# Running the first tile of expert 0 on batch 0's tokens while batch 1 is routed, and leaving the dummy matmuls out of the routing

## The reference

```python
# 1. windowed attention: 2 batches, 8 heads, 768 tokens, head size 64; keys 0..7 and the last 96 are kept
a = softmax(scale * q @ k.T - slope * dist, keep);  x = (a @ v) as [2, 768, 512]
# 2. mixture of 8 experts, one expert a token
for b in range(2):
    for s in range(768):
        fresh_e = argmax(x[b, s] @ w_gate)
        e = fresh_e if s == 0 or sigmoid(x[b, s] @ w_local) < 0.5 else prev_e
        prev_e = e
        out[b, s] = softmax(x[b, s] @ w_gate)[e] * (relu(x[b, s] @ w1[e]) @ w2[e])   # 512 -> 1024 -> 512
# 3. real part of a 2-D FFT of x added to x, layer norm, 512 -> 2048 -> 512 with relu, residual
```

## Time and profile before

| | |
|---|---|
| median of 3 timed runs | 678.57 us (677.31 to 679.86) |
| the profiled execution, its own time | 677.65 us |
| its span | 675.8 us |
| PE busy | 649.7 us, 96% of the span |
| VectorE, ScalarE, POOL busy | 317.0, 207.5, 213.7 us |
| share of PE in the chain that ended last | 85% |
| mean granted TensorE clock | 0.987 of full speed |

### The profile page before, as it was taken

One profiled execution on the slowest core, in us unless ns is written; L12 is line 12 of the kernel. 1 busy time (PEld: TensorE's weight loads), 2 busy tenths in 40 slices (PEclk: granted clock), 3 DMA queues, 4 the chain that ended last, 5 costly groups with the idle time before them and its releaser, 6 DMA issues.

```text
span 675.8 us, 10507 instructions
## 1 busy us (share of the span) xinstructions
PE 649.7 (96%) x3372; PEld 530.2 (78%) x3373; DVE 317.0 (47%) x828; ACT 207.5 (31%) x410; POOL 213.7 (32%) x120
## 2 busy tenths in 40 slices
PE   8999999769999999999998989999999999999997
PEld 7777878658888888888875668888888888888886
DVE  4999787574635446345347845441221111311112
ACT  3666544303332432433204752132211122111110
POOL 0000001235778777999515646270000000000000
PEclk9999999879999999999999989999999999999999
DMA  8664347226657556678255033210010000100001
GB/s 300 245 223 165 130 132 283 81 114 236 212 166 270 191 188 243 219 243 272 64 182 163 17 125 124 94 32 0 1 62 1 1 0 1 63 0 1 0 1 62
DMA packets 35409, 82.91 MB, mean 123 GB/s; under 512 B 3362, under 2 KB 7714, under 8 KB 35364
## 3 DMA queue, kind: packets, MB, share of 16 engines
q1 hardware_dynamic: 17952, 40.46, 16.8%
q10 hardware_dynamic: 15492, 35.56, 15.9%
q0 software_dynamic: 1920, 6.29, 2.8%
HBM read 67.35 MB, written 14.94 MB: 122 GB/s over the span
## 4 chain that ended last, share of the span: by engine, by line
PE 85%; DVE 9%; issue 2%; DMA 2%; ACT 1%; POOL 0%; DVEq 0%; ACTq 0%; POOLq 0%; SPq 0%
PE psum L597 22%; PE psum L599 22%; PE psum L598 22%; PE psum L1888 5%; PE psum L1860 3%; PE psum L1871 2%; PE psum L2036 2%; PE psum L1798 2%; PE psum L1996 1%; DVE prob L1407 1%; DMA bounds_i<-in_n_local 1%; PE psum L1792 1%; DVE prob_t L1421 1%; PE psum L2117 1%; DMA u<-y_sorted,result_rows 1%
## 5 line engine op out<-in xcount | busy, mean ns | idle before, releaser
L722 POOL TENSOR_TENSOR w<-raw,w 128x1024 fp32r<-128x1024 f32 x56 | 132.5, 2398 | 40.0 <-ACT w L820 39.8
L1752 DVE SCALAR_TENSOR_TENSOR act_t<-psum,act_t 128x512 fp32r<-128x512 f32 x48 | 33.2, 691 | 191.6 <-ACT act_t L1102 191.6
L820 ACT ACTIVATE w<-raw 128x1024 fp32r<-128x1024 f32 x64 | 67.3, 1058 | 123.9 <-PE psum L599 55.7
L1102 ACT ACTIVATE act_t<-psum 128x512 fp32r<-128x512 f32 x48 | 28.7, 598 | 217.8 <-PE psum L599 217.8
L597 PE MATMUL psum<-un_t,wc 128*128 128x512 f32 x192 | 75.5, 393 | 1.4 <-DVE un_t L1676 1.4
L597 PE MATMUL psum<-wc,act_t 128*128 128x512 f32 x192 | 75.6, 394 | 0.0
L599 PE MATMUL psum<-un_t,wc 128*128 128x512 f32 x192 | 75.4, 393 | 0.0
L598 PE MATMUL psum<-un_t,wc 128*128 128x512 f32 x192 | 75.2, 392 | 0.0
L599 PE MATMUL psum<-wc,act_t 128*128 128x512 f32 x192 | 74.8, 390 | 0.0
L598 PE MATMUL psum<-wc,act_t 128*128 128x512 f32 x192 | 74.8, 389 | 0.0
L874 ACT ACTIVATE prob<-prob,top 128x256 f32<-128x256 f32 (+1 forms) x96 | 46.2, 482 | 48.1 <-DVE top L1407 47.7
(11 more groups left out here) (273 smaller groups left out, 1109.9 us busy)
## 6 DMA issues: line engine op xcount, KB each, us to landing
raw<-in_moe_w ACTq DMA_DIRECT2D x60, 512.0 KB, 4.3
k_win<-in_k SPq DMA_DIRECT2D x8, 768.0 KB, 5.6
raw<-in_moe_w_ch SPq DMA_DIRECT2D x12, 512.0 KB, 3.3
v_win<-in_v SPq DMA_DIRECT2D x8, 704.0 KB, 4.2
xs<-x_sorted SPq DMA_DIRECT2D x17, 256.0 KB, 4.6
y_sorted<-ys SPq DMA_DIRECT2D x16, 256.0 KB, 3.4
q_t<-in_q SPq DMA_DIRECT2D x8, 384.0 KB, 3.5
out<-u SPq DMA_DIRECT2D x12, 256.0 KB, 2.0
```

The costliest lines, as they stand in the source:

```text
L722: nc.gpsimd.tensor_tensor(w[:, slot, 1, m, at_:at_ + PIECE], raw[:, n % RING, :], w[:, slot, 0, m, at_:at_ + PIECE].bitcast(f32), ALU.subt ...
L820: nc.scalar.activation(w[:, slot, 0, m, at_:at_ + PIECE], raw[:, n % RING, :], ACT.Copy).then_inc(high_done, 1)
L1102: nc.scalar.activation(act_t[n % 2][:, 0, :], bank(act_bank(n)), ACT.Relu).then_inc(act_high, 1)
L1752: nc.vector.scalar_tensor_tensor(act_t[n % 2][:, 1, :], bank(act_bank(n)), 0.0, act_t[n % 2][:, 0, :].bitcast(f32), ALU.max, ALU.subtract) ...
```

## The change

The first tile of the expert part is no longer "the first 128 tokens of expert 0", known once both batches are routed, but "the first tokens of batch 0 for expert 0, up to 128". They are known when batch 0 is routed, still during attention. `x_sorted` gets a block of 128 rows ahead of all areas for them; batch 0's scatter puts them there, and SP loads them as soon as batch 0's scatter is done. The remaining tokens of expert 0 begin a tile of their own. All the work of that tile then stands between the stages of batch 1's routing, and its first steps are done by ACT (`first_tile_high`, `first_tile_hidden`) and VectorE (`first_tile_low`, `first_tile_rest`) at fixed places. The 25 dummy matmuls around the routing are left out.

```diff
 # place(b), for b == 0
+link(tensor_scalar(in_first_tile, slot_f[:, these], 2.0 * P, float(P), ALU.is_lt, ALU.mult))
+link(tensor_tensor(slot_f[:, these], slot_f[:, these], in_first_tile, ALU.subtract))
 tensor_copy(slots[:, these], slot_f[:, these]).then_inc(slots_ready, 1)
 link(tensor_tensor(area, row["area"], upto[0][:, :, ST - 1], ALU.add))
+link(tensor_tensor(area, area, row["first_row"], ALU.max))
+link(tensor_tensor(sorted_first, area, row["first_row"], ALU.subtract))
 # control
-link(v.tensor_tensor_scan(last_tile, ones[:, 0:E], tiles, 0.0, ALU.mult, ALU.add))
+link(v.tensor_tensor_scan(last_tile, ones[:, 0:E], tiles, 1.0, ALU.mult, ALU.add))
 ...
 link(v.tensor_tensor(base_row[:, :], base_row[:, :], count[:, :], ALU.add))
+first_tile_rest()
 # ACT
+def first_tile_high():
+    act.wait_ge(xs_turned, 1)
+    activation(xs_t[0] high, bank(4), ACT.Copy).then_inc(xs_t_high, 1)
+def first_tile_hidden():
+    for part in range(2):
+        act.wait_ge(hid_sum, part + 3)
+        activation(hid[0][:, part * 512:(part + 1) * 512], bank(part), ACT.Relu).then_inc(hid_ready, 1)
+    act.wait_ge(hid_turned, 1)
+    for z in range(2):
+        activation(hid_t high, quarter z, bank(2 + z), ACT.Copy).then_inc(hid_t_high, 1)
 # DVE
+def first_tile_low():      dve.wait_ge(xs_t_high, 1);      xs_t[0] rest <- bank(4) - high
+def first_tile_rest():     for z in range(2): dve.wait_ge(hid_t_high, z + 1);  hid_t rest <- bank(2 + z) - high
+def first_tile_result():   dve.wait_ge(mm2_parts, 2 * PARTS);  ys[0] <- bank(5)
-x_tile(0, 0)
+x_tile(1, 1)
+first_tile_result()
 share(1)
 first_results()
-x_tile(1, 1)
-rectify(0, 0, 0)
-rectify(0, 0, 1)
-tile_step(0, 0, 2)
-mirrored_rows()
+x_tile(2, 0)
+rectify(1, 1, 0)
+rectify(1, 1, 1)
 tile_step(0, 1, 2)
+mirrored_rows()
 # SP
-sp.wait_ge(rows_ready, 1)
-first_rows = [row_of(j) for j in range(2)]
 sp.wait_ge(heads_cleared, 16)
 sp.wait_ge(results_cleared, 16)
-sp.wait_ge(scattered, 16 * NT)
-for par in range(2):
-    load_tile(first_rows[par], par)
+sp.wait_ge(first_scattered, 16 * ST)
+sp.dma_start(xs[0][:, :], x_sorted[0:P, :]).then_inc(xs_loaded[0], 16)
+sp.wait_ge(rows_ready, 1)
+first_rows = [row_of(j) for j in range(1, 3)]
+sp.wait_ge(scattered, 16 * ST)
+load_tile(first_rows[0], 1)
 sp.wait_ge(xs_turned, 1)
-load_tile(row_of(2), 0)
+load_tile(first_rows[1], 0)
 # PE, end of attention and routing of batch 1
-for t in range(4):
+for t in (2, 3, 0, 1):
     sum_last(t)
 values(UNITS - 1)
 turn_x(len(X_FILLS) - 1)
+turn_tile(0, 0, 16)
 for t in range(4, ST):
     sum_last(t)
-for stage in (turn_flags, ends_to_row, carry_to_column, codes_to_columns, rank_tokens): stage(1)
-pe.wait_ge(slots_ready, 2);  keep_busy(7)
-pe.wait_ge(rows_ready, 1);   keep_busy(8)
-pe.wait_ge(ctl_ready, 1);    half, odd = loads of ctl
-keep_busy(7)
-turn_tile(0, 0, 16)
-keep_busy(3)
-first_up(0, 0)
+pe.wait_ge(xs_t_ready, 1)
+up(0, 0, 0, 0, range(NC - 1));  turn_flags(1);  up(0, 0, 0, 0, range(NC - 1, NC))
+ends_to_row(1);  up(0, 0, 1, 0, range(1))
+carry_to_column(1);  codes_to_columns(1);  rank_tokens(1)
+up(0, 0, 1, 0, range(1, NC))
+for z in range(2): pe.wait_ge(hid_ready, z + 1); 4 transposes of hid[0]
+for c in range(NF - 2): second_product(0, 0, c)
+pe.wait_ge(ctl_ready, 1)
 turn_tile(1, 1, 16)
-up(0, 0, 1, slot_of(0))
+for c in range(NF - 2, NF): second_product(0, 0, c)
+first_up(1, 1);  half, odd = loads of ctl
+turn_tile(2, 0, 32)
+up(1, 1, 1, slot_of(1))
 mirror_rows()
-first_up(1, 1)
-tile_step(0, 0, 2)
+first_up(2, 0)
 tile_step(0, 1, 2)
```

More of the change, by code:

```diff
@@ L911, in _ @@
             act.wait_ge(ctl_ready, 1)
-            for n in range(2):
-                act.wait_ge(xs_loaded[n], 16)
+            act.wait_ge(xs_loaded[1], 16)
+            act.wait_ge(xs_loaded[0], 32)
             expert(1, 1)
@@ L1845, in rank_tokens, with keep_busy, turn_tile @@
                 nc.tensor.matmul(BANK_TOTALS, ones[:, :], flags, start=True, stop=True).then_inc(ranks_ready, 1)
+            def keep_busy(n):
+                for _ in range(n):
+                    nc.tensor.matmul(bank(7)[:, 0:2 * P], ident, square[:, 0:2 * P], start=True, stop=True)
+            def turn_tile(j, par, count):
+                pe.wait_ge(xs_loaded[par], count)
+                if not (isinstance(j, int) and j == 0):
+                    pe.wait_ge(xs_t_ready, j)
+                for c in range(NC):
+                    ins = nc.tensor.transpose(bank(4)[:, c * P:(c + 1) * P], xs[par][:, c * P:(c + 1) * P], ident)
+                ins.then_inc(xs_turned, 1)
@@ new lines, in ready_of, with slot_of, weights, up @@
+            def ready_of(j):
+                return nc.tensor.value_load(ctl[0:1, ds(j, 1)], min_val=0, max_val=(E - 1) * WPIECES)
+            def slot_of(j):
+                return nc.tensor.value_load(ctl[0:1, ds(SLOTS + j, 1)], min_val=0, max_val=1)
+            def weights(slot, x, m, c0):
+                return w[:, ds(slot, 1), x, m, c0:c0 + 512].rearrange("p s n -> p (s n)")
+            def up(j, par, part, slot, chunks=range(NC)):
+                if not (isinstance(j, int) and j == 0):
+                    pe.wait_ge(hid_ready, 2 * j + part - 1)
+                for c in chunks:
+                    c0 = c * F + part * 512
+                    ins = three_passes(bank(part), xs_t[par][:, 0, c, :], xs_t[par][:, 1, c, :],
+                                       weights(slot, 0, 0, c0), weights(slot, 1, 0, c0), c == 0, c == NC - 1)
+                if NC - 1 in chunks:
+                    ins.then_inc(hid_sum, 1)
@@ new lines, in tile_step @@
+            def tile_step(p, par, ahead):
+                j = 2 * p + par
+                early = isinstance(j, int)
+                if ahead == 0:
+                    keep_busy(1)
+                pe.wait_ge(hid_ready, 2 * j + 2)
+                if not (early and j == 0):
+                    pe.wait_ge(hid_t_ready, 2 * j)
+                for c in range(NF):
+                    ins = nc.tensor.transpose(bank(2 + c // 4)[:, (c % 4) * P:(c % 4 + 1) * P],
+                                              hid[par][:, c * P:(c + 1) * P], ident)
+                ins.then_inc(hid_turned, 1)
+                if ahead == 0:
+                    keep_busy(3)
+                if ahead >= 1:
+                    slot = slot_of(j + 1)
+                if ahead >= 2:
+                    up(j + 1, 1 - par, 1, slot)
+                    turn_tile(j + 2, par, 16 * p + 32)
+                if ahead == 1:
+                    up(j + 1, 1 - par, 1, slot, range(NC // 2))
+                own_slot = slot_of(j)
+                pe.wait_ge(rest_done, ready_of(j) + WPIECES)
+                if not (early and j < 2):
+                    pe.wait_ge(ys_ready, j - 1)
+                for c in range(NF):
+                    if c % 4 == 0:
+                        pe.wait_ge(hid_t_ready, 2 * j + c // 4 + 1)
+                    second_product(par, own_slot, c)
+                if ahead >= 2:
+                    first_up(j + 2, par)
+                if ahead == 1:
+                    up(j + 1, 1 - par, 1, slot, range(NC // 2, NC))
@@ new lines, in _ @@
+                turn_tile(0, 0, 16)
+            pe.wait_ge(rest_done, WPIECES // 2)
+            pe.wait_ge(xs_t_ready, 1)
+            up(0, 0, 0, 0, range(NC - 1))
+            turn_flags(1)
+            up(0, 0, 0, 0, range(NC - 1, NC))
+            ends_to_row(1)
+            up(0, 0, 1, 0, range(1))
+            carry_to_column(1)
+            codes_to_columns(1)
+            rank_tokens(1)
+            pe.wait_ge(rest_done, WPIECES)
+            up(0, 0, 1, 0, range(1, NC))
+            for z in range(2):
+                pe.wait_ge(hid_ready, z + 1)
+                for c in range(4):
+                    ins = nc.tensor.transpose(bank(2 + z)[:, c * P:(c + 1) * P],
+                                              hid[0][:, (4 * z + c) * P:(4 * z + c + 1) * P], ident)
@@ L2065, in mirror_rows @@
+            ins.then_inc(hid_turned, 1)
+            for c in range(NF - 2):
+                if c % 4 == 0:
+                    pe.wait_ge(hid_t_ready, c // 4 + 1)
+                second_product(0, 0, c)
+            pe.wait_ge(ctl_ready, 1)
             def mirror_rows():
```

180 lines of the change are left out of this document (84 added, 96 removed).

## The result

| | before | changed |
|---|---|---|
| median of 20 runs each | 677.65 us (676.12 to 679.86) | 683.96 us (675.75 to 686.26) |
| profiled execution, its span | 677.65, 675.8 us | 683.4, 681.6 us |
| mean granted TensorE clock | 0.987 | 0.980 |
| PE busy; share in the chain | 649.7 us; 85% | 644.3 us; 80% |

The ratio is 1.0069, with an interval of 1.0050 to 1.0088: 0.7% slower, where 669.0 and faster was forecast, and above the range, which ended at 674. The ratio compares the means of the fast runs, so the three slowest of the changed kernel's 20, which count as slow, are not in it. PE is busy 5.4 us less, but the dummies in the routing alone had been 13.1 us of its busy time.

What follows compares the result with a forecast made beforehand. PE was taken to bound the kernel, with holes set by batch 1's routing chain on VectorE. The terms put the second tile's transposes at 169.25 against 178.56, 9.3 us earlier, giving 669.0 us, range 665.5 to 674.

Steps and rivals of the forecast that it cites:

- Attention: Four small VectorE steps added by place(0) during attention: cost 0 if hidden, 0.85 us if not, taken as 0.3.
- First tile there in time: End of attention: the first tile's load arrives at 128.5, 0.7 us before PE turns it at 129.2; lateness taken as 0.
- Ready at 131.3 ... Nothing lost: After attention: the first tile's input is ready at 131.3, just when the gate sums come, at no cost.
- Flags +1.1, ranks +0.8: Batch 1's routing: flags wait 0.3 to 2.1 us behind nine matmuls, taken as 1.1; ranks reach VectorE 0.8 later.
- Control held 2.65: VectorE behind base_row: waits for the first tile's hidden values, done at ranks (R) + 5.6, holding control 2.65 us.
- Behind control 5.75: From control's end at 153.2 to the second tile's first product: 5.75 us of VectorE's steps, loads and input copies.
- Rival (b): VectorE's work behind control doesn't hold PE; first product 3.9 us earlier, saved 13.2, 665.1 us; chance 0.05.
- First product to transposes 9.2 + 0.8: Second tile, first product to hidden-value transposes: 9.2 us of PE's work, plus 0.8 for the clock.
- Dummies 0 to 3.3, taken as 0.8: Second tile's first products: low clock without dummies costs 0, 1.6 or 3.3 us; taken as 0.8.
- Rival (a): The low clock stays through the routing and again at 159: saved 4.9 us, 673.6; chance 0.14.
- rival (c): Experts' weights lead: POOL's row sets the pace from expert 1 on and starts 1.0 later; 679.6 us; chance 0.03.
- rival (d): Splitting expert 0 makes a 17th tile if batch 0 has under 68 tokens for it: 681.6 us; chance 0.03.

Runs made afterwards that it cites:

- e4: The kernel before, with its 25 dummy matmuls in the routing left out: ratio 0.9999 to the kernel before.
- e5: The kernel before, with VectorE's share(1) and first_results moved behind x_tile(1, 1): ratio 1.0195 to the kernel before.
- e2: The changed kernel, with PE's nine first products and VectorE's first four routing stages put ahead of the jump: ratio 1.0061 to the kernel before.
- e3: The changed kernel with 21 dummy matmuls put back: ratio 1.0000 to the kernel before.
- e8: e1 with the work ahead of the jump as in e2 and the 21 dummies of e3: ratio 0.9892 to the kernel before.
- e6: The changed kernel, both shares moved into VectorE's wait for ACT, place_results and first_results behind the second tile's input: ratio 0.9900 to the kernel before.
- e1: The changed kernel, with POOL's weight subtractions made to wait for the last step of first_results: ratio 0.9913 to the kernel before.
- e7: e6 with the work ahead of the jump as in e2 and the 21 dummies of e3: ratio 0.9881 to the kernel before.

## Why the prediction was wrong, point by point

The sum was 9.3 us sooner at the transposes; it was 5.1 later. The 14.4 us between are these:

- **Attention**: 0.7 (128.78 to 129.48), where 0.3 stood: 0.4 more, within its ends of 0 to 0.85. Executions of the other kernels differ by more than this (t0 from 128.86 to 134.34), so no part of it can be put down to the change.
- **First tile there in time**: right. SP's load was issued at 126.15, and the transposes follow the last turn without a wait.
- **"Ready at 131.3 ... Nothing lost", "nine matmuls start at 131.5"**: the input was ready at 131.7, but PE began at 134.16. The term that is missing is the jump. It was in the kernel before too, and could not be seen there: VectorE's 2.58 us ahead of the gate sums are put down to PE, and I took them for PE's. But PE's last sum had ended at 130.71 and VectorE began at 131.31, 0.6 later. In e4 and e5 it ended 1.0 ahead of VectorE's start, and VectorE's stop was 2.58 again (rows of e4 below): it was not PE that it waited for last. By e2, all of VectorE's 2.18 us go with the place of the instructions, and of PE's stop 2.3 us, with 1.07 left at the flags. The Trainium skill (Runtime: NRT & Kernel Launch, "Instruction fetch mechanics") says that a taken branch out of the window of fetched code makes the engine wait for it; e2 agrees with that as to place, but no run here shows the fetch itself.
- **Flags +1.1, ranks +0.8**: ranks came at 142.18, where 139.4 (with attention's 0.3) stood: 2.8 late, of which attention 0.4, the jump about 2, the rest the half clock on the nine products. They took 3.2 us (134.16 to 137.33), and 1.1 of wait was the middle between full and half. By e3, the clock alone is 1.0 there. So the 0.4 that I gave for a high clock in the small matmuls didn't come either: the flags' transpose took 0.42, against 0.27 in e3.
- **Control held 2.65**: it was held 4.0 (145.19 to 149.20). The way of it was right, but its nine products ran mostly at half clock, 3.7 us (141.93 to 145.66) for the 2.1 of the sum: with dummies (e8) the same hold is 2.5. (The terms of the R + 5.6 add up to 5.7, which changes nothing.)
- **Behind control 5.75**: 5.6. Right, the 1.3 for the two loads too. Rival (b) fails with it as long as the order is kept; e6, with another order, has the first product 2.4 us behind control, 3.3 sooner.
- **First product to transposes 9.2 + 0.8**: 20.7. This is the step that failed: 10.7 of the 14.4. The sum counted PE's work there and nothing of VectorE's. The change moves `share(1)` and `first_results` from ahead of `x_tile(1, 1)` to behind it; I costed this edit at nothing and didn't name what hides it. In the kernel before they ended at 158.34, and POOL began at 158.60. What stood there were six steps of 12.2 us together beside POOL's subtractions, for which PE waited 7.6 us and then ran twelve products at half clock. e1 prices it: 9.5 of the 10.7 go with one wait. Of what is left, 0.7 is the half clock at the first twelve products beyond the 0.8 of the sum; the last 0.5 is not traced.
- **Dummies 0 to 3.3, taken as 0.8**: the twelve products at 162.91 took 4.2 us and the twelve at 178.70 took 4.8, where 2.75 each stood, so the price was 3.5, a little over the upper end. 2.0 of it hang on the wait of 7.6 us and are gone in e1. All that the dummies brought in e3 is 4.7 us of time, because the low clock also stretched the hold of control and pushed VectorE into POOL's time. Rival (a) had its mechanism right, and alone would have given 673.6.
- **Weights, rival (c)**: don't lead, as said (e1). **A 17th tile, rival (d)**: 16 stores. None of the rivals had two engines in each other's way, and all of the slower side was given to (d).

Timelines of VectorE and PE in e4, for the stop at the jump in a kernel like the one before:

```profile
136.57 0.21 DVE L1179 TENSOR_TENSOR logits<-psum,logits_part 128x54 f32<-128x54 f32 x1 [2.58 <-PE psum L1798]
134.96 0.61 PE L1798 MATMUL psum<-gate_w,x_t 128*128 128x9 f32 x4 [0.47 <-ACT x_t L851]
```

The contention could have been read. The kernel before shows a step stretched beside POOL, in VectorE's timeline:

```profile
176.87 2.36 DVE L1300 COPY p_sel<-by_token 128x6 f32<-128x6 f32 x1
179.14 0.15 DVE L1302 COPY p_sel<-psum 128x6 f32<-128x6 f32 x1
```

The copy from SBUF takes 2.36 us and ends at 179.23, POOL's six subtractions end at 179.20; its neighbour from PSUM takes 0.15.

## What to carry to other kernels

When an edit moves small VectorE steps, look at what GpSimd runs at their new place: beside back-to-back GpSimd work, count up to a whole GpSimd instruction for each of them (2.33 us here), not its own 0.2 us, unless it is of a kind that was not held, and ask who is queued behind. A wait of one engine on another is the place for such steps, and a long hole in front of one engine's work (a jump, here) can lie unseen under a wait that the profile puts down to another. Dummy matmuls that cost and bring nothing can begin to matter when the change gives TensorE real work there; they belong ahead of the work whose price is the clock, not between two pieces of the path (the last six of e7).

## What the runs showed of the hardware

- **Small steps of VectorE were held until a running GpSimd instruction ended.** With GpSimd subtracting 128 x 1024 in 2.33 us, VectorE's TENSOR_SCALAR, CAST, COPY and TENSOR_TENSOR with all inputs in SBUF took 1.5 to 2.5 us for 0.16 to 0.25 (changed kernel, e3, e5; the COPY in the kernel before), each ending 0.03 to 0.15 us behind the end of one subtraction, if these are taken as equally long. GpSimd was not slowed: its eight took 18.63 us beside six held steps, 18.89 in e1 beside none. TENSOR_REDUCE (0.20 at 167.33 in the changed kernel) and RECIPROCAL stayed at 0.19 to 0.20, and steps with an input in PSUM at their usual length (0.68 for 128 x 512). The Trainium skill (SBUF — State Buffer, "Who interferes with whom") gives as rule that the two share a pair of ports which one instruction holds to its end, that reductions never take it, and that copies, casts and scalar steps can, if their operands meet certain conditions, as does a step with two inputs in SBUF. The rows agree in each of these kinds. That the steps were held from outside and not slow by themselves is shown by e1 and e5; that it is these ports is the page's word.
- **The same step can be short or long by a few tenths of a microsecond.** In e3 POOL began at 163.58: the multiplication at 163.11 was over by then and took 0.25 us, the one at 163.63 took 2.36. In the changed kernel, where POOL had begun, both were long (2.13 and 2.04).
- **The clock at half was cheap for one kernel and 0.7% for another** (e4, e3), by what PE had on the path at that time.
- **A stop behind the jump.** Behind the end of the conditional block VectorE stood still for 2.2 to 2.5 us and PE for 2.9 to 3.2 (changed kernel, e1, e6). It went from VectorE with work placed ahead of the jump (e2); what is behind it, no run shows.
